# Starting w2's and h's buffers at multiples of 2048 bytes in an attention and mixture-of-experts kernel

## What is computed

```python
scores = np.where(mask, q @ k.T / 8, -1e9)          # mask: 0 <= rel < 64
x = (softmax(scores) @ v) as [2304, 512]
P = np.exp(x @ w_gate - (x @ w_gate).max())
for _ in range(8):
    P /= P.sum(1, keepdims=True) + 1e-09
    P /= P.sum(0, keepdims=True) + 1e-09
    P *= N / E
for e in range(E):
    out += P[:, e:e + 1] * (np.maximum(x @ w1[e], 0.0) @ w2[e])
```

## Time and profile before

| | |
|---|---|
| time, median of 3 runs | 1596.03 us (1595.70 to 1596.58) |
| profiled execution | 1596.36 us |
| its span, first to last instruction | 1594.6 us |
| TensorE busy | 1577.8 us, 99% |
| TensorE weight loads busy | 1426.9 us, 89% |
| GpSimd busy | 991.3 us, 62% |
| VectorE busy | 693.6 us, 43% |
| ScalarE busy | 543.7 us, 34% |
| moved by DMA | 120.44 MB, 76 GB/s |

### The profile page before, as it was taken

How to read it: one execution, slowest core, us unless ns; L and a number is a source line. 1 busy time by engine, 2 the same in 40 slices (tenths; PEclk the granted TensorE clock), 3 DMA queues, 4 the chain that set the end, 5 groups by cost and what they waited for, 6 DMA issues and landing times.

```text
span 1594.6 us, 24053 instructions
## 1 busy us (share of the span) xinstructions
PE 1577.8 (99%) x8886; PEld 1426.9 (89%) x8886; DVE 693.6 (43%) x1262; ACT 543.7 (34%) x785; POOL 991.3 (62%) x642
## 2 busy tenths in 40 slices
PE   7999999999999999999999999999999999999999
PEld 6889889999999999999999999998999999999998
DVE  5844543443443434434434434434344344344343
ACT  4743242333333343333323233333323333232331
POOL 4985555656565876656565565878556565656652
PEclk9999999999999999999999999999999999999999
DMA  7621212121221213122121212113121211212111
GB/s 219 184 82 54 80 54 79 53 80 56 76 76 56 79 53 119 53 80 69 63 79 53 79 53 79 65 66 118 55 80 53 79 58 73 79 53 79 53 66 39
DMA packets 34159, 120.44 MB, mean 76 GB/s; under 512 B 3904, under 2 KB 4160, under 8 KB 34112
## 3 DMA queue, kind: packets, MB, share of 16 engines
q1 hardware_dynamic: 34112, 119.80, 21.9%
HBM read 115.06 MB, written 4.72 MB: 75 GB/s over the span
## 4 chain that ended last, share of the span: by engine, by line
PE 92%; POOL 6%; DVE 1%; issue 1%; ACT 1%; DVEq 0%; POOLq 0%; ACTq 0%
PE ps L496 16%; PE ps L494 16%; PE ps L495 16%; PE ps L457 14%; PE ps L455 14%; PE ps L453 14%; POOL probs L843 2%; POOL xv_lo L829 1%; POOL sc L835 1%; POOL w_lo L801 1%; POOL w_raw L835 0%; POOL w_lo L808 0%; PE ps L539 0%; PE ps L374 0%; ACT w_hi L580 0%
## 5 line engine op out<-in xcount | busy, mean ns | idle before, releaser
L801 POOL TENSOR_TENSOR w_lo<-w_raw,w_hi 128x1792 fp32r<-128x1792 f32 (+2 forms) x97 | 387.3, 3993 | 532.5 <-ACT w_hi L580 532.5
L635 ACT ACTIVATE h_hi<-ps 128x384 fp32r<-128x384 f32 x384 | 186.2, 491 | 867.5 <-DVE ps L983 430.1
L496 PE MATMUL ps<-w_hi,h_lo 128*128 128x512 f32 x1152 | 451.3, 392 | 0.0
L494 PE MATMUL ps<-w_hi,h_hi 128*128 128x512 f32 x1152 | 448.8, 390 | 0.0
L457 PE MATMUL ps<-xv_hi,w_lo 128*128 128x384 f32 x1330 | 448.3, 337 | 0.0
L495 PE MATMUL ps<-w_lo,h_hi 128*128 128x512 f32 x1152 | 448.2, 389 | 0.0
L453 PE MATMUL ps<-xv_hi,w_hi 128*128 128x384 f32 x1330 | 445.3, 335 | 1.0 <-DVE h_lo L957 0.7
L455 PE MATMUL ps<-xv_lo,w_hi 128*128 128x384 f32 x1330 | 445.9, 335 | 0.0
L957 DVE SCALAR_TENSOR_TENSOR h_lo<-ps,h_hi 128x384 fp32r<-128x384 f32 x384 | 205.6, 555 | 269.6 <-ACT h_hi L635 261.0
L455 PEld LDWEIGHTS ps<-xv_lo,w_hi 128*128 128x128 f32 x1330 | 249.7, 188 | 17.5
L453 PEld LDWEIGHTS ps<-xv_hi,w_hi 128*128 128x128 f32 x1330 | 249.8, 188 | 17.2 <-DVE h_lo L957 2.4
(11 more groups left out here) (98 smaller groups left out, 964.6 us busy)
## 6 DMA issues: line engine op xcount, KB each, us to landing
w_raw<-w SPq DMA_DIRECT2D x192, 512.0 KB, 3.9
qk_buf<-qk SPq DMA_DIRECT2D x16, 576.0 KB, 5.9
v_win<-v SPq DMA_DIRECT2D x16, 288.0 KB, 4.5
out<-x_raw SPq DMA_DIRECT2D x18, 256.0 KB, 4.4
const_sb<-consts SPq DMA_DIRECT2D x1, 176.0 KB, 3.6
wg<-w_gate SPq DMA_DIRECT2D x1, 64.0 KB, 3.7
```

Of the source, the lines that this page charges most:

```text
L494: nc.tensor.matmul(ps_y[t], h_hi[slot][:, f, c], w2_hi[slot][:, f, :], start=opens, stop=False)
L496: last = nc.tensor.matmul(ps_y[t], h_lo[slot][:, f, c], w2_hi[slot][:, f, :], start=False, stop=closes)
L635: nc.scalar.activation(h_hi[slot][:, f, half * HT:(half + 1) * HT], o, ACT.Relu)\
L801: last = nc.gpsimd.tensor_tensor(w1_lo[:, slot, c], w1_raw[:, slot, (lo + 1) * BLK:(hi + 1) * BLK], w1_hi[:, slot, c].bitcast(F32), ALU.su ...
```

## The change

The declarations of four small tiles trade places. max_diag (512 bytes of a partition) moves from the end of the layout to the front, where col_part, max_part and max_all (32 bytes each with the rounding) were; those three go to the end. Sizes, uses and instructions stay as they are. All tiles that are declared behind const_sb get a start 416 bytes further on.

```diff
         wg = sb(ctx, "wg", [P, KT, GC])
-        col_part = sb(ctx, "col_part", [P, E])
-        max_part = sb(ctx, "max_part", [P, 1])
-        max_all = sb(ctx, "max_all", [P, 1])
+        max_diag = sb(ctx, "max_diag", [P, P])
         ones = sb(ctx, "ones", [P, P])
         const_sb = sb(ctx, "const_sb", [P, WINDOW + 2 * P + GC])
         w2_hi = [sb(ctx, "w2_hi0", [P, 2, DM], F32R)]
...
         logits = sb(ctx, "logits", [P, NT, E])
         prob = sb(ctx, "prob", [P, NT, E])
-        max_diag = sb(ctx, "max_diag", [P, P])
+        col_part = sb(ctx, "col_part", [P, E])
+        max_part = sb(ctx, "max_part", [P, 1])
+        max_all = sb(ctx, "max_all", [P, 1])
```

## The result

| | before | after |
|---|---|---|
| time, median | 1595.87 us (4 runs, 1595.31 to 1596.58) | 1608.47 us (4 runs, 1607.79 to 1608.54) |
| span of the profiled execution | 1594.6 us | 1606.7 us |
| one window (28 in a row) | 15.520 us | 15.653 us |

The ratio is 1.0075, with a 95% interval of 1.0062 to 1.0088: slower by 12.6 us, where no change was forecast.

A forecast was written before the change was run, and what follows sets the result against it. TensorE's matmul spacing was taken to bound the kernel from 103 us on. 1594.6 us of span plus nothing plus 1.76 us gave 1596.36; the runs' median, 1596.03, was taken as forecast, predicted 1596.0, range 1593.0 to 1598.0.

The forecast's parts named there:

- The frame: Whole kernel: from 103 us on only the spacing of TensorE's matmuls counts; the edit changes only starts in SBUF.
- the wide matmuls' moving operand: Second product's reads of w2: moving their start ends crossings of 2048 multiples, worth at most 0.4 us, taken as 0.
- the one on the coarser grid: Starts of w2 and h at multiples of 64 rather than 32 bytes: buys nothing, 0.
- a cost of crossings: Reads of w2 across a multiple of 2048 bytes: below 0.12 ns a crossing, from equal 15.520 us windows.
- the gap: No trace row shows a stream starting at multiples of 512 or 2048; given the first rival's chance, 5%.
- the wrong rival, a gain: Wide matmuls: aligned starts remove their 13.0 ns excess, 45 us gained, 1551 us; chance 5%.
- the term for places in the sum: Effect of the moved starts in SBUF on the kernel's time: put at 0.
- the collision: Aligned w2 and h: a weight load and the stream beside it slow each other, up to 47 us, 1643 us; chance 5%.
- the branch that I had priced lowest: Slowing only where h's first piece follows xv, a few times a window: under 4 us in all.
- decision point: Weight loads beside wide matmuls: slowing shows once a load of 188 ns takes over 226.
- the signs that I had named: Changed kernel's trace: window 15.52 us, wide starts 0.226 us apart, loads 188 ns, score steps 1151 and 2110 ns.
- The 13 ns excess: Wide and narrow matmuls: 13.0 and 13.8 ns above one column a cycle, going with the matmul, not its address.

The follow-up runs named there:

- first416: Kernel before with 416 unused bytes ahead of x_raw, so all buffers move together and w2 and h start at multiples of 2048: 1596.3 us, ratio 0.9999.
- c_pad416: Kernel before, small tiles not exchanged, with 416 unused bytes behind const_sb, so w2, h and all behind start as in the changed kernel: 1608.8 us, ratio 1.0081.
- all1664: Kernel before with 32 unused bytes behind const_sb, w2 and h together at 1664 modulo 2048: 1603.8 us, ratio 1.0048.
- all1760: Kernel before with 128 unused bytes behind const_sb, w2 and h together at 1760 modulo 2048: 1603.1 us, ratio 1.0039.
- w2_0_h_96: Kernel before with unused bytes that put w2's buffers at multiples of 2048 and h's at 96 past one: 1613.8 us, ratio 1.0113.
- bench: Kernel's computation replaced by matmuls alone, weights 0 to 224 bytes from their stream: wide spacing 0.2267 us at 0, up to 0.2342 at others.
- bench2: Like bench, matmuls alone, but consecutive streams start at two places in turn: 231.5 ns a step at 0 and 64 with weights at the other's place.

## Why the prediction was wrong

**The frame was right.** From 103 us on only the spacing of matmuls counts; the other engines, the transfers, the loads at 188 to 189 ns and attention's steps (1153 and 2113 ns on sc) stayed, the small tiles cost nothing, and the edit did put the starts where I worked them out to be.

**The step that failed** is "the wide matmuls' moving operand", with the one on the coarser grid behind it. The three lengths of a window in the earlier trace rows are equal, and I took that as the price of a start's place. But xv's four starts, 1152, 640, 128 and 1664, are all 128 modulo 512: they differ in crossing a multiple of 2048 and in nothing else. The test could rule out a cost of crossings, and did (first416 and c_pad416 read w2 without a crossing, one at before's time and one at after's). It could say nothing of the places modulo 256, by which the edit moved w2 and h against xv and w1: from 224 to 128. I named the gap ("no row shows a stream whose starts are multiples of 512 or 2048") and tied it to the wrong rival, a gain. So the term for places in the sum, put at 0, left out the change of distance, which measured 12.6 us.

**The rival that came true** was the collision, in the branch that I had priced lowest: "only those against xv and w1 do" change, "under 4 us in all". The mechanism was there in part: a load and a stream that meet, by their distance. The condition that I gave it, w2 and h both on a grid of 512, was wrong: first416 has them there at before's time, and all1664 and all1760 lose 7 to 8 us without it. And the term was mis-sized. I charged one matmul a few times a window with 14 ns. It is eight switches, each disturbing about six matmuls, 17 ns in sum. The measured 0.133 us a window was to be had from no row of before; but its own 0.07 us between the window (15.520) and 42 x 0.1738 + 36 x 0.2263 us pointed to a cost of the switches, and so to something that could grow.

**Its decision point was wrong too.** I let it decide once a load passes 226 ns. Loads stayed at 188 ns and the steps grew all the same: w2_0_h_96 has 234 ns a step with loads of 188 to 189. Of the signs that I had named, the window alone moved; the steady wide spacing and the loads stood, because I had looked for the loss in each matmul and not behind the switches. The Trainium skill ("SBUF — State Buffer", "Who interferes with whom") lists TensorE's two read ports as independent and lets PE wait on no one; bench disagrees, with 226.7 ns at equal starts and 229.0 to 234.2 at others and no other engine at work.

**The 13 ns excess** I had tied to the matmul and not to its address. That held: no layout and no part of the two benches had a steady spacing below 226.7 and 173.3 ns. Both are 13.3 ns above one column a cycle; my 13.0 and 13.8 differed by the rounding of short stretches. What the 13.3 ns are stays open. Open as well is what in the memory repeats after 256 bytes, why a stream needs some six matmuls to settle (in bench the stream at 96 takes nine, 122.19 to 124.28 us, at 232 ns), and why the switches' cost over the distance is not the same in bench (33 ns for two at 0, 96, 128 and 160) as in the kernel. Open too is which reads meet when streams change place (bench2). Only 4-byte operands were tried.

## What to carry to other kernels

Where 4-byte matmuls run back to back with new weights each, let the weights and their moving operand start at the same place modulo 256 bytes, and try the distance between two products that take turns; alignment to a round address by itself bought nothing. An exchange of small tiles ahead of large ones moved this kernel by 0.8%, and 32 bytes between w2 and h by 1.4%, so compare layouts by their starts, not by their code. A natural experiment in a trace counts only for what really differs in it: write down all residues before reading "no effect" from it.

## What the runs showed of the hardware that was not expected

- Two reads of TensorE meet: 226.7 ns a wide matmul with the weights at the stream's start modulo 256, 229.0 to 234.2 ns at 32 to 224 bytes from it, with all other engines idle. The rule is for streams that keep their place: taking turns at 0 and 64 with the weights all at 64 runs at 226.7, and with each load at the place of the stream beside it at 231.5.
- A start by itself has no price: multiples of 2048 (first416) and 96 past them (the second fence of bench) run alike.
- At the start of bench the first wide matmuls come 0.427 us apart (nine steps from 20.42 to 24.26 us), what 512 columns take at 1.2 GHz, with no excess at all; the excess appears with the fast spacing. The view's granted clock reads 1.00 there, so this rests on the spacing alone.
